# Start addresses of the matmul operands moved to multiples of 512 bytes, in a gated-attention kernel with two expert layers

## The chip, the core and the metric

The kernel runs on one core of a Trainium2 chip. The metric is device time in microseconds (us) of one execution, as the median of several; lower is better. The core has TensorE (PE, matmuls), VectorE (DVE), ScalarE (ACT), GpSimd (POOL), and SyncE (SP), whose queue issues the DMAs here. On-chip memory (SBUF) has 128 partitions, and a tensor in it starts at the same byte address in each of them; matmul results go to PSUM, in eight banks.

## The reference

A gated linear attention makes x, a bilinear layer follows, then a mixture of four experts:

```
state = alpha[t][:, None] * state + k[t] (outer) v[t];  y[t] = q[t] @ state      # 4 batches, 8 heads, 768 steps, D = 48
x = y as [3072 tokens, 384]
x = ((x @ w1) * (x @ w2)) @ w3 @ w_out                                           # 384 -> 1024 -> 384
p = domain_probs / (sum(domain_probs) + 1e-9)
out = sum over e of p[:, e] * (relu(x @ w1e[e]) @ w2e[e])                        # 4 experts, 384 -> 1024 -> 384
```

## The kernel before

Matrices are float32. A product is made from three float32r matmuls: each operand is split into a high part (a copy rounded to float32r, by ACT) and a low part (what the rounding left, by DVE or POOL), and high*high, high*low and low*high are added in PSUM. The program has three stages.

The fold (from the start to about 60 us) multiplies w3 by w_out once, `wp = w3 @ w_out`, with plain float32 matmuls of 384 columns (lines 1132 and 1147), while the first chunks of the attention are worked on beside it.

The bilinear stage (about 60 to 430 us) runs over 4 batches, two tiles of 384 tokens in each and 8 steps of 128 features in a tile. A step makes `a` and `b` from the tile `x0` and the weights `wb` (`up1`), multiplies them to `g` (DVE), and adds `g @ wp` into three PSUM banks (`down1`); all of it goes through `split_product` (lines 940 to 942), which is 27 matmuls of 384 columns in a step and 1728 in the stage. Its moving operand (the one that is streamed, the other being loaded into the array beforehand) is `x0`, read as three pieces of 128 columns that lie 4096 bytes apart, or `g`, read as one piece. Beside the steps, PE works on the attention of the next chunk (`visit`), DVE prepares the one after it, and SP moves data: the keys are turned by way of memory (`keys_spill`, lines 312 and 320) and a part of x0 is moved between partitions (`move_rest`, line 355), for which PE waits on `x0_moved` before the first step of a tile. The result `x1` is written to memory.

The expert stage (about 430 to 1230 us) is 4 experts times 3 rounds times 16 steps, 192 steps. A step is 9 matmuls of 512 columns (`up2_product`, line 1089: moving `x1`, loaded `we`) laid among 12 of 384 columns (`down2_product`, line 1198: moving `we`, loaded `h`), 4032 matmuls in the stage with a few less at its edges. ACT writes `h_hi` and DVE `h_lo` from the PSUM bank that a step filled, two steps ahead of their use.

The order on every engine is written out by hand, and waits are on semaphores.

SBUF tensors are laid out one behind the other, in the order in which the program names them (the helper `sb`); each starts at the next multiple of 32 bytes, and the first of the kernel's own at byte 1152. Tensors named with the context `first` are given back at `first.close()`, and those behind it (x1, we1, total) start again where the first of them (`inputs`) did. So these starts follow:

| tensor | role in the matmuls | start before (bytes) | over a multiple of 512 | start after | over |
|---|---|---|---|---|---|
| h_hi, h_lo | loaded, line 1198 | 3552, 7648 | 480 | 4096, 8192 | 0 |
| x1 tiles (four) | moving, line 1089 | 11968 and on | 192 | 12288 and on | 0 |
| inputs | attention | 11968 | 192 | 12288 | 0 |
| keys_t, values | attention | 46784, 40640 | 192 | 47104, 40960 | 0 |
| decayed, scores | attention | 49600, 50656 | 448, 480 | 49920, 50944 | 256 |
| wb, we1 (and low) | loaded or moving | 54752 and on | 480 | 55296 and on | 0 |
| wp (and low) | loaded, `down1` | 103904 and on | 480 | 104448 and on | 0 |
| x0 tiles (two) | moving, `up1` | 128480, 140768 | 480 | 129024, 141312 | 0 |
| a, g (and parts) | moving (g) | 153056 and on | 480 | 153600 and on | 0 |
| we0, w3 | loaded or moving | 174560 | 480 | 175104 | 0 |

Slices of the weights that a matmul reads start at multiples of 512 bytes from the tensor's start. Every start is a multiple of 32 bytes, before and after; those at 192 are multiples of 64 too, those at 480 are not.

Of the kernel before, what the change touches and what calls it, by code (L numbers as in the profile page):

```python
# [24 lines left out]
F32 = mybir.dt.float32  # L25
F32R = mybir.dt.float32r
# [4 lines left out]
P = 128  # L31
BATCH, HEADS, SEQ, D = 4, 8, 768, 48
CHUNK = P
CHUNKS = SEQ // CHUNK
PAIRS = HEADS // 2
# [8 lines left out]
KT, FT = DM // P, FF // P  # L44
# [9 lines left out]
TILE2 = 512  # L54
# [24 lines left out]
TURNED = CHUNKS - 1  # L79

ATTENTION_COLUMNS = (SLOTS * 3 + 2 + 2 + 2 + 1) * PAIRS * CHUNK + SLOTS * VD + PAIRS * P + PAIRS * D + PAIRS * ODD + 2 * PAIRS
ATTENTION_REST = ATTENTION_COLUMNS - 4 * KT * TILE2
REDO_X0 = 2 * CHUNKS


def gated_attention_experts(nc, akq, v, akq_long, v_columns, w3T, w_out, wsets, probs, out):
# [4 lines left out]
    with ExitStack() as ctx:  # L91
        def sb(name, shape, dt=F32, where=ctx):
            return where.enter_context(nc.sbuf_tensor(name, shape, dt))
# [13 lines left out]
        gate = sb("gate", [P, TOKENS // P, EXPERTS])  # L107
        gate_sum = sb("gate_sum", [P, TOKENS // P])
        gate_inv = sb("gate_inv", [P, TOKENS // P])
        h_hi = sb("h_hi", [P, 2, TILE2], F32R)  # L110
        h_lo = sb("h_lo", [P, 2, TILE2], F32R)
        outside = sb("outside", [PD, BATCH * CHUNKS])
        outside_sum = sb("outside_sum", [1, 1])
        regular = sb("regular", [1, 1], mybir.dt.int32)
        head_sum = sb("head_sum", [PD, 2])
        alpha_range = sb("alpha_range", [PD, 2])


        first = ExitStack()
# [7 lines left out]
        keys_t = sb("keys_t", [P, PAIRS, P], F32, first)  # L127
        state = sb("state", [PD, PAIRS, D], F32, first)
        decayed = sb("decayed", [PD, PAIRS, ODD], F32, first)
        chunk_decay_inv = sb("chunk_decay_inv", [PD, 2, PAIRS], F32, first)  # L130
        scores = sb("scores", [P, 2, PAIRS, CHUNK], F32, first)

        wb_hi = sb("wb_hi", [P, WSET], F32R, first)
        raw = ExitStack()
# [27 lines left out]
        for slot in range(2):  # L162
            x1_hi[slot] = sb(f"x1_{slot}_hi", [P, KT, TILE2], F32R)
            x1_lo[slot] = sb(f"x1_{slot}_lo", [P, KT, TILE2], F32R)
        sb("attention_rest", [P, ATTENTION_REST])
        we_hi[1] = sb("we1_hi", [P, WSET], F32R)
# [1119 lines left out]
```

## Time and profile before

| | |
|---|---|
| median of 3 runs | 1230.63 us (1230.1 to 1231.71) |
| the profiled execution's own time | 1231.72 us |
| its span (first to last instruction) | 1230.0 us |
| mean granted TensorE clock | 1.00 of full speed |
| busy: PE, PEld, DVE, ACT, POOL | 99%, 91%, 36%, 22%, 14% of the span |
| DMA | 107.49 MB, 87 GB/s over the span |

PE is the matmul side of TensorE, PEld the loading of its stationary operand. Matmuls are pipelined: the record of one lasts longer than the distance to the next one's start, so the cost of a matmul in a stream is read as the distance between starts, or as a stretch divided by the matmuls that start in it. The queue of SP is shown as SPq.

### The profile page before, as it was taken

To read this page: it belongs to the slowest core of one execution; us is meant where nothing else is said; L and a number is where in the kernel's file an instruction comes from. 1 tells how busy PE (TensorE), PEld (TensorE's weight loads), DVE (VectorE), ACT (ScalarE), POOL (GpSimd) and SP (SyncE) were. 2 spreads that over 40 slices of the span, in tenths; PEclk is the share of its full clock that TensorE was granted. 3 is DMA by queue.
4 is the path that set the end of the run, shared out by engine and by line. 5 is a ranking of instruction groups with operands and counts; after the bars stand their busy time and mean duration, and the time that the engine had idled before them with its cause. 6 is when DMAs were issued, how large, how long until landed. Compare 5 with 4: busy or idle time off the path is not lost.

```text
span 1230.0 us, 18716 instructions
## 1 busy us (share of the span) xinstructions
PE 1218.8 (99%) x7714; PEld 1114.2 (91%) x7714; DVE 446.6 (36%) x873; ACT 276.0 (22%) x515; POOL 168.1 (14%) x148
## 2 busy tenths in 40 slices
PE   9998999999999999999999999999999999999999
PEld 6698999999999999999999999999999999999998
DVE  4876765765741122222222222221222222222222
ACT  1433333333332321111111111111111111111111
POOL 1122222222222630000000000000000000000000
PEclk9999999999999999999999999999999999999999
DMA  9634635635622440111141111113011111222201
GB/s 274 214 77 106 144 104 121 144 106 119 139 58 110 142 166 28 51 51 52 52 155 52 52 51 51 52 51 132 25 50 51 52 52 52 78 77 77 77 4 48
DMA packets 81639, 107.49 MB, mean 87 GB/s; under 512 B 36001, under 2 KB 54689, under 8 KB 81057
## 3 DMA queue, kind: packets, MB, share of 16 engines
q1 hardware_dynamic: 81568, 106.50, 28.9%
q8 instruction: 51, 0.84, 0.3%
q14 instruction: 20, 0.16, 0.1%
HBM read 86.03 MB, written 18.09 MB: 85 GB/s over the span
## 4 chain that ended last, share of the span: by engine, by line
PE 91%; DVE 4%; DMA 2%; SPq 2%; issue 1%; ACT 1%; DVEq 0%; ACTq 0%
PE bank L1089 32%; PE bank L1198 24%; PE score_banks L1198 8%; PE bank L940 7%; PE bank L942 6%; PE bank L941 6%; PE bank L1132 2%; PE bank L1147 1%; PE bank L979 1%; PE bank L989 1%; DMA keys_t<-keys_spill 1%; PE score_banks L1000 1%; SPq L320 1%; DMA keys_spill<-key_blocks 1%; DVE suffix L687 1%; PE score_banks L965 1%
## 5 line engine op out<-in xcount | busy, mean ns | idle before, releaser
L764 DVE SCALAR_TENSOR_TENSOR h_lo<-bank,h_hi 128x512 fp32r<-128x512 f32 x192 | 132.7, 691 | 584.7 <-ACT h_hi L558 583.8
L558 ACT ACTIVATE h_hi<-bank 128x512 fp32r<-128x512 f32 x192 | 114.7, 597 | 661.4 <-PE bank L1089 661.4
L1089 PE MATMUL bank<-x_hi,we_lo 128*128 128x512 f32 x576 | 228.7, 397 | 0.0
L1089 PE MATMUL bank<-x_hi,we_hi 128*128 128x512 f32 x576 | 224.1, 389 | 0.0
L1089 PE MATMUL bank<-x_lo,we_hi 128*128 128x512 f32 x576 | 223.5, 388 | 0.0
L1198 PE MATMUL bank<-we_hi,h_hi 128*128 128x384 f32 x576 | 194.6, 338 | 0.0
L1198 PE MATMUL bank<-we_lo,h_hi 128*128 128x384 f32 x576 | 194.5, 338 | 0.0
L1198 PE MATMUL bank<-we_hi,h_lo 128*128 128x384 f32 x576 | 193.8, 336 | 0.0
L461 POOL TENSOR_TENSOR we_lo<-we_raw,we_hi (+1 forms) x48 | 60.9, 1291 | 527.6 <-ACT we_hi L519 527.6
L940 PE MATMUL bank<-x,wb_hi 128*128 128x384 f32 x384 | 128.8, 335 | 3.6 <-DMA x<-x 2.3
L1089 PEld LDWEIGHTS bank<-x_lo,we_hi 128*128 128x128 f32 x576 | 108.3, 188 | 22.7
L1089 PEld LDWEIGHTS bank<-x_hi,we_lo 128*128 128x128 f32 x576 | 108.3, 188 | 22.4
L942 PE MATMUL bank<-x,wb_lo 128*128 128x384 f32 x384 | 128.4, 334 | 0.0
L941 PE MATMUL bank<-x,wb_hi 128*128 128x384 f32 x384 | 128.3, 334 | 0.0
L1198 PEld LDWEIGHTS bank<-we_hi,h_lo 128*128 128x128 f32 x576 | 108.3, 188 | 8.5
L1198 PEld LDWEIGHTS bank<-we_hi,h_hi 128*128 128x128 f32 x576 | 108.3, 188 | 8.4
L1089 PEld LDWEIGHTS bank<-x_hi,we_hi 128*128 128x128 f32 x576 | 108.3, 188 | 0.2
L1198 PEld LDWEIGHTS bank<-we_lo,h_hi 128*128 128x128 f32 x576 | 108.1, 188 | 0.0
L471 POOL TENSOR_TENSOR g_lo<-g_sb,g_hi 128x384 fp32r<-128x384 f32 x64 | 65.5, 1023 | 233.2 <-ACT g_hi L548 233.2
L940 PEld LDWEIGHTS bank<-x,wb_hi 128*128 128x128 f32 x384 | 72.1, 188 | 4.7 <-DMA x<-x 2.9
L754 DVE TENSOR_TENSOR g_sb<-a_sb,bank 128x384 f32<-128x384 f32 x64 | 35.2, 551 | 105.6 <-PE bank L942 103.0
L941 PEld LDWEIGHTS bank<-x,wb_hi 128*128 128x128 f32 x384 | 72.1, 188 | 0.0
(89 smaller groups left out, 1434.8 us busy)
## 6 DMA issues: line engine op xcount, KB each, us to landing
x_hi<-x_hi_spill SPq DMA_DIRECT2D x24, 768.0 KB, 4.8
x_lo<-x_lo_spill SPq DMA_DIRECT2D x24, 768.0 KB, 6.4
inputs<-akq SPq DMA_DIRECT2D x24, 672.0 KB, 5.5
we_raw<-wset SPq DMA_DIRECT2D x4, 3072.0 KB, 10.1
values<-v_rows SPq DMA_DIRECT2D x24, 256.0 KB, 5.8
x_hi_spill<-x_hi_out SPq DMA_DIRECT2D x8, 576.0 KB, 3.4
x_lo_spill<-x_lo_out SPq DMA_DIRECT2D x8, 576.0 KB, 4.4
keys_spill<-key_blocks SPq DMA_DIRECT2D x60, 64.0 KB, 1.8
```

Of the source, the lines that this page charges most:

```text
L320: sp.dma_start(keys_t[:, pair, :].rearrange("p (i e) -> p i e", i=BLOCKS), rows[:, :, pair * BLOCK:(pair + 1) * BLOCK]).then_inc(keys_t_lo ...
L461: pool.tensor_tensor(set_lo(n)[:, at], set_raw(n)[:, at], set_hi(n)[:, at], ALU.subtract).then_inc(piece_lo, 1)
L471: pool.tensor_tensor(g_lo[:, s % 2, :], g_sb[:, s % 2, :], g_hi[:, s % 2, :], ALU.subtract).then_inc(g_lo_ready, 1)
L558: act.activation(h_hi[:, s % 2, :], bank[s % 2][:, :], ACT.Relu).then_inc(h_hi_ready, 1)
L754: dve.tensor_tensor(g_sb[:, s % 2, :], a_sb[:, s % 2, :], bank[1][:, 0:TILE1], ALU.mult).then_inc(g_ready, 1)
L764: dve.scalar_tensor_tensor(out=h_lo[:, s % 2, :], in0=bank[s % 2][:, :], scalar=0.0, in1=h_hi[:, s % 2, :], op0=ALU.max, op1=ALU.subtract) ...
L940: pe.matmul(dst, left[0], right[0], start=first, stop=False)
L941: pe.matmul(dst, left[0], right[1], start=False, stop=False)
L942: return pe.matmul(dst, left[1], right[0], start=False, stop=last)
L1089: mm = pe.matmul(bank[s % 2][:, :], (we_hi if term < 2 else we_lo)[e % 2][:, cols], (x1_lo if term == 1 else x1_hi)[u][:, k, :], start=(i ...
L1132: mm = pe.matmul(bank[FOLD_BANKS[f]][:, 0:DM], w3_sb[:, k, f * P:(f + 1) * P], wo_sb[:, k, :], start=(k == 0), stop=(k == FT - 1))
L1198: mm = pe.matmul(bank[SUM_BANKS[sub]][:, 0:DM], (h_hi if term < 2 else h_lo)[:, s % 2, rows], (we_lo if term == 1 else we_hi)[e % 2][:, cols],
```

## The change

Two tensors that nothing reads are put in as padding, `edge_of_h` (320 bytes in each partition) and `edge_of_weights` (224 bytes). h_hi and h_lo are named behind the five small tensors that they stood ahead of, and `chunk_decay_inv` (32 bytes) behind `scores`. `attention_rest`, the space kept between x1 and we1, is 224 bytes longer so that we1 still lies on wb. Every instruction, wait, shape and DMA, and the order on each engine, is the same as before; only addresses in SBUF differ. All tensors of the table move; the highest byte used in a partition goes from 223712 to 224256.

```diff
 ATTENTION_COLUMNS = (SLOTS * 3 + 2 + 2 + 2 + 1) * PAIRS * CHUNK + SLOTS * VD + PAIRS * P + PAIRS * D + PAIRS * ODD + 2 * PAIRS
-ATTENTION_REST = ATTENTION_COLUMNS - 4 * KT * TILE2
+EDGE_OF_H, EDGE_OF_WEIGHTS = 80, 56
+ATTENTION_REST = ATTENTION_COLUMNS + EDGE_OF_WEIGHTS - 4 * KT * TILE2
...
         gate_inv = sb("gate_inv", [P, TOKENS // P])
-        h_hi = sb("h_hi", [P, 2, TILE2], F32R)
-        h_lo = sb("h_lo", [P, 2, TILE2], F32R)
         outside = sb("outside", [PD, BATCH * CHUNKS])
...
         alpha_range = sb("alpha_range", [PD, 2])
+        sb("edge_of_h", [P, EDGE_OF_H])
+        h_hi = sb("h_hi", [P, 2, TILE2], F32R)
+        h_lo = sb("h_lo", [P, 2, TILE2], F32R)
...
         decayed = sb("decayed", [PD, PAIRS, ODD], F32, first)
+        scores = sb("scores", [P, 2, PAIRS, CHUNK], F32, first)
         chunk_decay_inv = sb("chunk_decay_inv", [PD, 2, PAIRS], F32, first)
-        scores = sb("scores", [P, 2, PAIRS, CHUNK], F32, first)
+        sb("edge_of_weights", [P, EDGE_OF_WEIGHTS], F32, first)
```

## Rows read from the trace of the kernel before

**Rows 1.** The page's head: busy time of each engine over the span.
```profile
span 1230.0 us, 18716 instructions
PE 1218.8 (99%) x7714; PEld 1114.2 (91%) x7714; DVE 446.6 (36%) x873; ACT 276.0 (22%) x515; POOL 168.1 (14%) x148
```

**Rows 2.** Windows; columns: stretch, length, engines, granted clock, DMA share, GB/s.
```profile
60.00:150.00 90.00, 84.56 (x832) 80.56 (x831) 66.09 (x150) 31.00 (x64) 23.54 (x21) 1.00 0.44 101
250.00:350.00 100.00, 99.06 (x920) 95.77 (x919) 63.77 (x144) 33.51 (x68) 25.86 (x24) 1.00 0.48 114
600.00:800.00 200.00, 200.00 (x1012) 182.31 (x1011) 47.53 (x73) 34.91 (x60) 15.23 (x12) 1.00 0.18 63
```

**Rows 3.** Timeline of PE, expert stage, one step; columns: start, record's length, instruction.
```profile
700.13 0.39 PE L1089 MATMUL bank<-x_hi,we_hi 128*128 128x512 f32 x1
700.36 0.34 PE L1198 MATMUL bank<-we_hi,h_hi 128*128 128x384 f32 x1
700.54 0.39 PE L1089 MATMUL bank<-x_lo,we_hi 128*128 128x512 f32 x1
...
704.29 0.39 PE L1089 MATMUL bank<-x_hi,we_hi 128*128 128x512 f32 x1
```

**Rows 4.** Timeline of PE, bilinear stage: first with g, then with x0 moving.
```profile
299.53 0.33 PE L941 MATMUL bank<-g_lo,wp_hi 128*128 128x384 f32 x1
...
300.40 0.33 PE L940 MATMUL bank<-x,wb_hi 128*128 128x384 f32 x1
...
303.17 0.33 PE L941 MATMUL bank<-x,wb_hi 128*128 128x384 f32 x1
```

**Rows 5.** The chain that ended last, in the fold: start, length, what.
```profile
19.35 3.24 PE bank L1132 x10
22.60 0.59 PE score_banks L965 x14
```

**Rows 6.** Groups of PE by line and shape: busy us, mean ns of one record, idle.
```profile
L1089 PE MATMUL bank<-x_hi,we_lo 128*128 128x512 f32 x576 | 228.7, 397 | 0.0
L1089 PE MATMUL bank<-x_hi,we_hi 128*128 128x512 f32 x576 | 224.1, 389 | 0.0
L1089 PE MATMUL bank<-x_lo,we_hi 128*128 128x512 f32 x576 | 223.5, 388 | 0.0
...
L1198 PE MATMUL bank<-we_hi,h_hi 128*128 128x384 f32 x576 | 194.6, 338 | 0.0
...
L942 PE MATMUL bank<-x,wb_lo 128*128 128x384 f32 x384 | 128.4, 334 | 0.0
...
L941 PE MATMUL bank<-g_lo,wp_hi 128*128 128x384 f32 x192 | 64.2, 334 | 0.0
```

**Rows 7.** Waits of PE for other engines and DMAs: us in total, times, longest.
```profile
PE score_banks L965 <- DMA keys_t<-keys_spill: 3.0, 4, 1.5
PE bank L940 <- DMA x<-x: 2.3, 1, 2.3
PE bank L940 <- DVE g_sb L754: 1.3, 1, 1.3
```

**Rows 8.** The chain that ended last, up to the longest of these waits.
```profile
100.23 1.80 DMA keys_spill<-key_blocks
...
104.17 1.66 SPq L320
...
105.87 2.24 SPq L355
...
108.15 2.22 DMA x<-x
...
110.41 0.44 PE bank L940
```

**Rows 9.** DMA issues: count, KB each, median us to landing.
```profile
x_hi<-x_hi_spill SPq DMA_DIRECT2D x24, 768.0 KB, 4.8
...
keys_t<-keys_spill SPq DMA_DIRECT2D x60, 64.0 KB, 4.5
...
x<-x SPq DMA_DIRECT2D x48, 48.0 KB, 2.8
```

## The prediction

> **What bounds the kernel.** I read the page's head first: PE is busy 99% of a span of 1230.0 us, DVE 36%, ACT 22% [rows 1]. A busy PE can still stand in line for data, so next come the waits of PE: all that it waited for others is 3.0 + 2.3 + 1.3 = 6.6 us, 0.5% of the span [rows 7]. The windows say the same by stage: 200.00 busy of 200.00 among the experts, 99.06 of 100.00 in the bilinear stage, 84.56 of 90.00 between 60 and 150 us, all at a granted clock of 1.00, which is the 2.4 GHz level [rows 2]. So the kernel is a stream of matmuls, and a change that leaves every instruction in place can act in two ways only: on the distance between the starts of two matmuls, or on those 6.6 us of waits (with small stalls behind them, which add little).
>
> **What a matmul costs.** In the expert stage a step goes from 700.13 to 704.29, 4.16 us for 9 matmuls of 512 columns and 12 of 384 [rows 3]. After a start with 512 columns the next comes 0.23 us later, after one with 384 0.18 us later: 128 columns more cost some 0.05 us, one column in each cycle at 2.4 GHz. By that rate the columns of a step take 9 x 213.3 + 12 x 160 = 3840 ns, and 4160 - 3840 = 320 ns is on top, 15 ns for each of 21 matmuls. The window gives the same: 200 us over 1012 starts is 197.6 ns, the columns are 3840 / 21 = 182.9, 14.7 ns on top [rows 2]. In the bilinear stage, with x0 moving, 16 distances take 303.17 - 300.40 = 2.77 us, 173.1 ns each, 13 on top of 160; with g moving 5 take 0.87 us, 174 each, 14 on top [rows 4]. The float32 matmuls of the fold start 10 times in 22.60 - 19.35 = 3.25 us, 325 ns each (the step to the next kind counted in); that is two cycles for each column, 320, and at most 5 ns on top [rows 5]. So a float32r matmul pays 13 to 15 ns beyond its columns, a float32 one 5 or less. Over 1728 + 4032 matmuls this is 1728 x 13 + 4032 x 14.7 = 82 us. That is all that the operands' addresses could possibly have to do with on PE, and it is what has to be judged.
>
> **The change part by part.** It removes and adds no instruction and moves none past another, so each part is a new address and its price is what that address does.
>
> (a) The moving operand. Before there were three cases. x1 stood 192 bytes over a multiple of 512; we and g 480 over; x0 480 over too, but read in three pieces, so it would meet a bad start three times where g meets it once. They cost the same: x0 13 ns, g 14 ns on top [rows 4], and the mean records of x0 and g are both 334 ns [rows 6]. x1, with 64-byte alignment, has 230 - 213 = 17 ns behind it at the two digits of the timeline, and no less than we has [rows 3]. If a start off 512 cost one more fetch, three pieces would pay three times; they pay nothing. Price taken: 0. From both sides: at best the 13 to 15 ns fall to the 5 ns of the fold (a gain of 8 x 1728 + 9.7 x 4032 = 53 us), at worst a matmul pays what separates the dearest row of its kind from the cheapest, 397 - 388 = 9 ns (rival 3). I take 0 because the nearest rows, x0 against g, differ in just what would matter and agree.
>
> (b) The loaded operand (h, we, wb, wp). All of these stood 480 over before, 32 bytes off a multiple of 64, so no row here shows an aligned one. This is the weak place. What speaks for 0: the time on top is the same 13 to 15 ns under 384 and under 512 columns [rows 3, 4], so it isn't a load that ends too late, which 53 ns more of columns would cover. What speaks against: float32 loads stood 480 over too (w3) and show 5 ns or less [rows 5], but there the columns take twice as long and could hide a loss. Price taken: 0, with the same ends as in (a).
>
> The Trainium skill, "SBUF — State Buffer" (box on SBUF cachelines in the section on the DMA port swizzle), says that engines read lines of 16 bytes. All starts before and after are multiples of 16, so by that rule nothing changes on PE, though it leaves the 13 ns unexplained and no row here shows such a line.
>
> (c) DVE, ACT, POOL. Their operands move in the same way. DVE matters only from 60 to 110 us, where it is behind part of the chain; over the span it has 64% of slack [rows 1]. Nothing in the trace ties its times to an address. 0.
>
> (d) DMAs. Their SBUF ends move from 192 or 480 over to 0. Only two kinds are waited for: keys_t, 3.0 us in four waits, and x<-x, 2.3 us in one [rows 7]. In the longest wait, the chain runs through a spill of 1.80 us, the queue of SP (1.66 us and 2.24 us are two of its pieces) and an x<-x of 2.22 us [rows 8], so about 4 us of 10 are transfers. Most of such a transfer is not data: 48 KB land after 2.8 us where 768 KB land after 4.8 [rows 9], so (768 - 48) KB cost 2.0 us and 48 KB of data only 0.13 us, the rest being fixed. Were the data part of the transfers a fifth cheaper, a chain of two or three would gain under 0.1 us; with keys_t in four waits I take 0.3 us in all. The ends: 0, and all 5.3 us of waits for DMA gone; and +1 us if the order of landings falls worse. The ends of x1, we and inputs are hidden: PE has no wait for them in the list.
>
> The Trainium skill, "DMA: Bandwidth & Descriptors" (How a descriptor splits into AXI transactions), speaks for a gain: a piece that doesn't start at a multiple of 256 bytes fetches from the boundary below it. By it a 1024-byte piece of x0 at 480 over costs 39 beats, and 32 at 0, an estimate of 18% less; on the 0.13 us of data that is 0.02 us, on a whole landing of 2.2 us 0.4 us. No row here has an aligned DMA to hold against it, and the sum above goes without it.
>
> **The sum.** 0 on PE, 0.3 us less on DMA waits. The profiled execution took 1231.72 us for a span of 1230.0, 1.7 us around it, and lies 1.1 us above the median of 1230.63. Taken from its own time, 1231.7 - 0.3 = 1231.4; against the median, 1230.3. I give 1230.3.
>
> **The rivals.**
> 1. The time on top is an alignment loss of float32r, and it goes. All of it down to the fold's 5 ns gives 1230.6 - 53 = 1177; if only the loaded operand counts in one of the two kinds, or half is left, about 1204. For it: float32 matmuls don't have it [rows 5], and no loaded operand was aligned. Against it: x0 in three pieces equals g in one [rows 4, 6], and x1 at 192 is no better than we at 480 [rows 3]. A loss that comes only from the loading side is still open. Chance 0.12.
> 2. The waits for DMA shrink enough to be seen: more than 2.5 us of their 5.3. Their whole goes to 1225.3; half gives 1228. For it: the transfers stand on the chain [rows 8]. Against: they are mostly fixed time [rows 9], and SP's queue stands between them. Chance 0.05.
> 3. Slower: two reads, or a read and a write, in step. Before, x1 stood 192 over and h and we 480 over, so that the up matmul's stream and the load of the next h beside it began in different places modulo 512; afterwards all begin in the same. Where such a meeting costs time, line 1089 shows it: its third kind already has a record of 397 ns against 388 and 389 for the others [rows 6], at the same shape, so something does cost 8 to 9 ns there. If the other two kinds take that price, 2 x 576 x 8.5 = 10 us are added, 1240. Against: x0 with wb, and we with h, were in step before (all 480 over) and have the lowest times on top. It decides from the mean of those two rows: at 392 it would be some 4 us. Chance 0.09.
> 4. Something slower of 2.5 us or more from the early part, DMA landings that fall worse for SP's queue: the waits of [rows 7] grow by half, 1233.9. Chance 0.04.
> The forecast, no change, has 0.70. That the change doesn't do what it says is no rival here: the starts in the table follow from the sizes of the tensors.
>
> **How the numbers follow.** The bound of 0.2% is 2.5 us, about what a measurement of this kernel can tell from no change; three runs lay 1.6 us apart. Faster is rivals 1 and 2, 0.17; slower rivals 3 and 4, 0.13; same 0.70. The forecast's own range is 1228.2 to 1233.1. To leave out no more than 2 in 10 the range takes in rival 2 down to its end, 1225, and rival 3 up to 1240; what is left out is mostly rival 1 (0.12), which lies far below.
>
> **What would show it.** In the profile after: a step of the expert stage again 4.16 us long, and 1012 starts in 600 to 800 us, one more or less; if rival 1 holds, 1012 becomes above 1030 and the distances of 173 ns fall toward 165. Line 1089's three rows should stay at 397, 389 and 388; rival 3 lifts the lower two. The bilinear window should keep its 920 starts. The waits of PE should be 6.6 us within 1 us, with x<-x still there. I am wrong if the distance between float32r matmuls moves by as little as half a nanosecond: over 5760 of them that is 2.9 us.

## The result, and the profile after

The kernel after takes 1244.15 us (median of 5, 1243.47 to 1245.33) against 1230.1 us before (5, 1228.65 to 1231.71); the ratio of the runs on record is 1.0102, 95% interval 1.0086 to 1.0118 (the two medians alone give 1.0114, inside it). It is slower by 1%. The forecast was 1230.3 us, no change, with a range up to 1240: it was wrong. The span went from 1230.0 to 1241.9 us.

The page of the kernel after, its head:

```profile
span 1241.9 us, 18716 instructions
PE 1232.7 (99%) x7714; PEld 1119.0 (90%) x7714; DVE 446.3 (36%) x873; ACT 276.1 (22%) x515; POOL 168.2 (14%) x148
```

PE alone has grown, 1218.8 to 1232.7 us; DVE, ACT and POOL are the same within 0.3 us [rows 1]. The window of the expert stage in the kernel after (columns as in [rows 2]):

```profile
600.00:800.00 200.00, 200.00 (x993) 180.16 (x992) 44.95 (x69) 34.31 (x59) 15.28 (x12) 1.00 0.18 63
```

Among the experts 993 matmuls fit where 1012 did [rows 2], at the same granted clock of 1.00. The timeline of PE in the kernel after shows a step from 700.65 to 704.89, 4.24 us, against 4.16 [rows 3]; line 1092 is line 1089 of before:

```profile
700.65 0.39 PE L1092 MATMUL bank<-x_hi,we_hi 128*128 128x512 f32 x1
700.88 0.34 PE L1201 MATMUL score_banks<-we_hi,h_lo 128*128 128x384 f32 x1
701.06 0.40 PE L1092 MATMUL bank<-x_lo,we_hi 128*128 128x512 f32 x1
701.29 0.34 PE L1201 MATMUL bank<-we_hi,h_hi 128*128 128x384 f32 x1
...
704.89 0.39 PE L1092 MATMUL bank<-x_hi,we_hi 128*128 128x512 f32 x1
```

What is loaded beside each stream is in the same timeline, in the rows of PEld:

```profile
700.65 0.19 PEld L1201 LDWEIGHTS score_banks<-we_hi,h_lo 128*128 128x128 f32 x1
700.88 0.19 PEld L1092 LDWEIGHTS bank<-x_lo,we_hi 128*128 128x128 f32 x1
701.06 0.19 PEld L1201 LDWEIGHTS bank<-we_hi,h_hi 128*128 128x128 f32 x1
```

A load starts together with the matmul before its own: at 700.65 and 701.06 x1 is streamed and h is loaded, at 700.88 the weights are streamed and weights are loaded. Where two down matmuls follow each other, the weights are streamed and h is loaded. In a step of this order no weights are loaded beside a stream of x1.

The groups of PE after (mean ns of a record before the last bar):

```profile
L1092 PE MATMUL bank<-x_hi,we_lo 128*128 128x512 f32 x576 | 229.2, 398 | 0.0
L1092 PE MATMUL bank<-x_lo,we_hi 128*128 128x512 f32 x576 | 229.2, 398 | 0.0
L1092 PE MATMUL bank<-x_hi,we_hi 128*128 128x512 f32 x576 | 224.6, 390 | 0.0
...
L1201 PE MATMUL bank<-we_hi,h_hi 128*128 128x384 f32 x576 | 195.5, 339 | 0.0
...
L945 PE MATMUL bank<-x,wb_lo 128*128 128x384 f32 x384 | 128.4, 334 | 0.0
```

The row of x_lo went from 388 to 398 ns, the level that x_hi,we_lo had already; the others rose by 1; the bilinear rows stayed at 334 [rows 6]. Records hide part of it, distances between starts do not. Their means over the stage's steps, worked out from all starts in the two traces (D a down matmul of 384 columns, U0, U1, U2 the up matmuls with x_hi,we_hi, with x_lo and with we_lo):

| from > to | D>D | D>U0 | U0>D | D>U1 | U1>D | D>U2 | U2>D | sum, x 3 = a step |
|---|---|---|---|---|---|---|---|---|
| before, ns | 174.2 | 175.0 | 226.7 | 180.0 | 225.8 | 172.5 | 232.5 | 4160 |
| after, ns | 175.8 | 181.7 | 229.2 | 175.8 | 237.5 | 175.8 | 237.5 | 4240 |

They repeat to 1 ns from step to step, but for a few distances where the stage begins and ends, whichever of four experts, three values of k and eight of f the matmul is for. So nothing random is at work in these two kernels, and nothing that hangs on where in a tensor a matmul reads, which changes in steps of 512 bytes or more. Nor is it the writing of h: ACT and DVE write it in 0.6 and 0.7 us of a step's 4.2, while the distances are alike in all three thirds of a step. The two ends of the stage, first from the timeline of before, then of after:

```profile
426.42 0.39 PE L1089 MATMUL bank<-x_hi,we_hi 128*128 128x512 f32 x1
...
1226.57 0.34 PE L1198 MATMUL bank<-we_hi,h_lo 128*128 128x384 f32 x1
```

```profile
423.20 0.39 PE L1092 MATMUL bank<-x_hi,we_hi 128*128 128x512 f32 x1
...
1238.53 0.34 PE L1201 MATMUL bank<-we_hi,h_lo 128*128 128x384 f32 x1
```

The expert stage takes 815.33 us instead of 800.15, 15.2 us more, which is 192 steps of 79 ns. It begins 3.2 us earlier. 15.2 - 3.2 = 12.0, the growth of the span. These are two single executions, and single ones of one kernel lie 2 to 3 us apart; with the medians the kernel lost 14.05 us, so the early part gave back 1.1 us of the 15.2, and with the recorded ratio 2.7 us (0.7 to 4.6 by its interval). The waits of PE after, against [rows 7], hold 2.1 of the 3.2 us:

```profile
PE score_banks L968 <- DMA keys_t<-keys_spill: 1.8, 1, 1.8
PE bank L943 <- DMA x<-x: 1.4, 1, 1.4
PE bank L943 <- DVE g_sb L757: 1.3, 1, 1.3
```

### The profile page after: what moved, and what is told of

Read it like the earlier page. It is cut to its first block, busy times and chain, and to the rows that moved or that the text cites. A ratio compares the mean times of both kernels' runs of the same rounds, so it can differ in the third digit from the quotient of the medians.

```text
span 1241.9 us, 18716 instructions
## 1 busy us (share of the span) xinstructions
PE 1232.7 (99%) x7714; PEld 1119.0 (90%) x7714; DVE 446.3 (36%) x873; ACT 276.1 (22%) x515; POOL 168.2 (14%) x148
## 4 chain that ended last, share of the span: by engine, by line
PE 95%; DVE 3%; SPq 1%; DMA 1%; ACT 0%; issue 0%; DVEq 0%
PE bank L1092 33%; PE bank L1201 25%; PE score_banks L1201 8%; PE bank L943 8%; PE bank L945 7%; PE bank L944 7%; PE bank L1135 2%; PE bank L982 2%; PE bank L1150 1%; PE score_banks L1003 1%; PE bank L992 1%; PE score_banks L968 1%; DVE wb_lo L773 0%; DVE suffix L690 0%; DVE decay L711 0%
## 5 line engine op out<-in xcount | busy, mean ns | idle before, releaser
L1092 PE MATMUL bank<-x_hi,we_lo 128*128 128x512 f32 x576 | 229.2, 398 | 0.0
L1092 PE MATMUL bank<-x_lo,we_hi 128*128 128x512 f32 x576 | 229.2, 398 | 0.0
```

The source lines that it names most:

```text
L1092: mm = pe.matmul(bank[s % 2][:, :], (we_hi if term < 2 else we_lo)[e % 2][:, cols], (x1_lo if term == 1 else x1_hi)[u][:, k, :], start=(i ...
```

## The experiments

Theory A: the price depends on how x1 stands to h and to the weights modulo some length. Theory B: it depends on each start by itself. All kernels but the two named up384, which leave out a quarter of the tokens of the expert stage, compute the whole result. x1_224 and x0_g_224, taken on two chips with the same starts of x1, h and the weights, have the same seven distances to 0.1 ns, so one profile of a kernel is enough for those; it is not enough for 1 or 2 us in the whole time. Each of the first group is the kernel after with other paddings; `edge_of_x1` is a third padding, between h_lo and the attention's inputs:

```diff
-EDGE_OF_H, EDGE_OF_WEIGHTS = 80, 56
+EDGE_OF_H, EDGE_OF_X1, EDGE_OF_WEIGHTS = 80, 56, 0        # x1_224; all_480: 72, 0, 56; h_w_288: 24, 56, 0
...
         h_lo = sb("h_lo", [P, 2, TILE2], F32R)
+        sb("edge_of_x1", [P, EDGE_OF_X1])
```

**all_480.** 

> h, x1 and the weights all start 480 bytes over a multiple of 512 (before: h and weights 480, x1 192; after: all 0). Theory A, in step: what costs the 80 ns in each expert step (4.16 to 4.24 us) is that x1 now starts at the same place modulo 512 as h and the weights, wherever that is. It expects this kernel to be like the one after: 992 or 993 matmul starts in 600 to 800 us, some 1244 us. Theory B, the place itself: weights or h at 0 over are dear and at 480 over cheap. It expects 1012 starts and some 1230 us.

Measured: 1246.5 us, ratio to before 1.0126 (1.0108 to 1.0143), a step of 4.24 us, and each of the seven distances as after, within 0.1 ns. Its window:

```profile
600.00:800.00 200.00, 200.00 (x993) 180.14 (x992) 45.64 (x69) 34.32 (x59) 15.30 (x12) 1.00 0.17 59
```

None of x1, h and the weights starts at a multiple of 64 bytes in it. Theory B falls for h and the weights, which stand where they stood before. That x1's own start could be dear, at 480 as at 0, is not excluded here; h_w_288 below does that, with x1 at 0 and a step of 4.16 us.

**x1_224.** 

> The kernel after, with x1 (and the attention's inputs, which share its start) moved 224 bytes further, so that x1 stands to the weights and h as it did before, but these stay at 0 over. Theory A (only the relation counts): 1012 starts in 600 to 800 us, a step of 4.16 us, 1230 us. Theory B (weights and h at 0 are dear by themselves): 993 starts, 4.24 us, 1244 us.

Measured: 1230.47 us, ratio 0.999 (0.998 to 1.0), 4.16 us a step, the seven distances those of before. One tensor's place undoes the whole loss.

```profile
600.00:800.00 200.00, 200.00 (x1011) 182.20 (x1010) 47.77 (x73) 34.91 (x60) 15.23 (x12) 1.00 0.18 63
```

**The other places of x1.** One profile and one time each (0 and 224 are the kernels above, with their medians). The attention's tensors, which are not in use in the expert stage, move along.

> As x1_224 but x1 only 32 bytes over, weights and h at 0. 224 and 32 are the same modulo 64. Theory A with a period of 64 bytes: the same as x1_224, 4.16 us a step. Theory A with a longer period: a third value. Theory B: 4.24 us.

> As x1_224 but x1 64 bytes over, weights and h at 0. Theory A with a period of 64 bytes or less: like the kernel after, 4.24 us a step, 993 starts. With a longer period: some other value, perhaps 4.16. Theory B: 4.24 us.

> The kernel after, x1 at 128 over, weights and h at 0. With x1 at 32, 64 and 224 over the step was 4.17, 4.18 and 4.16 us. A fixed loss only where the starts are equal expects 4.16 to 4.18 here; a loss that repeats every 128 bytes expects 4.24.

> The kernel after, x1 at 256 over, weights and h at 0. The steps were 4.24 (0), 4.17 (32), 4.18 (64), 4.19 (128) and 4.16 us (224). A loss that repeats every 256 bytes expects 4.24; one that fades with the distance expects 4.16 to 4.18.

> The kernel after, x1 at 96 over, weights and h at 0. Theory P: the loss has a period of 256 bytes and one peak, at equal starts (4.24 us at 0 and 256), and is flat elsewhere: 4.16 to 4.19 us a step. Rival Q: it also has peaks between, in which case some of 96, 160 and 192 reach 4.2 or more. For the bilinear stage: it has ended at 422 to 424 us wherever the attention's inputs started at 0, 32, 64, 128 or 256 over and at 425 or later at 192, 224 and 480; I expect 424 here.

> As x1_96, x1 at 160 over. Theory P: 4.16 to 4.19 us a step. Rival Q: 4.2 or more at one of the three. Bilinear stage: 425 if the late end goes with starts in the upper half of 256 bytes, else 423.

> As x1_96, x1 at 192 over. This differs from x1_224 (4.16) by one step of 32 bytes. Theory P: 4.16 to 4.18 us a step. Rival Q: 4.2 or more at one of the three. Bilinear stage: 426, as before, where the inputs stood at 192 too.

Measured, with h and weights at 0 over (the step is the trace's distance over ten steps, divided by ten):

| x1 over 512 | 0 (after) | 32 | 64 | 96 | 128 | 160 | 192 | 224 | 256 |
|---|---|---|---|---|---|---|---|---|---|
| step, ns | 4240 | 4170 | 4180 | 4200 | 4190 | 4200 | 4200 | 4160 | 4240 |
| U1>D, ns | 237.5 | 230.0 | 232.5 | 231.5 | 234.2 | 232.5 | 231.6 | 225.8 | 237.5 |
| whole time, us | 1244.15 | 1230.64 | 1231.99 | 1235.57 | 1235.23 | 1237.26 | 1237.16 | 1230.47 | 1242.62 |
| first up matmul at, us | 423.2 | 423.5 | 423.0 | 422.7 | 424.3 | 424.4 | 424.3 | 426.6 | 422.2 |

At 256 all seven distances are those of 0: a shift by 256 bytes changes nothing there, and each smaller shift does. Whether the other places repeat 256 bytes on was not tried. In x1_32 and x1_128 the distances change in turn from step to step (4168 and 4172, 4186 and 4194 ns), and the table has the means. Equal starts are the dearest place, 40 ns above the next, but the rest isn't flat: the expected 4.16 to 4.19 was too narrow, three places have 4.20, which just meets what rival Q asked. The kernel of before stood, by chance or not, at the best of the eight. The first up matmul, expected at 424, 423 or 425, and 426 us for 96, 160 and 192 over, came at 422.7, 424.4 and 424.3.

**h_288 and w_288.** 

> The kernel after, with h_hi and h_lo alone moved, to 288 over a multiple of 512, so that x1 stands 224 bytes past h modulo 512 as it did before; x1 and the weights stay at 0 over. Theory A1: what counts is the stream of x1 in an up matmul against h, which is loaded beside it for the next down matmul; a step of the expert stage falls back to about 4.16 us, span some 1230. Theory A2: what counts is x1 against the weights; the step stays at 4.24 us. Something between means that both count.

> The kernel after, with all weights, x0 and g moved together to 288 over, so that x1 stands 224 bytes past the weights as before; h and x1 stay at 0 over. Theory A1 (x1 against h): 4.24 us a step. Theory A2 (x1 against the weights): 4.16. It also sets h against the weights for the first time: what the down matmuls pay for being in step would show as another distance between two down matmuls (175.8 ns after, 174.2 before).

Measured: 4220 and 4200 ns (1239.12 and 1236.31 us, one time each). Neither kernel gives back all of the 80 ns: one gives 20, the other 40. D>D, where no x1 takes part, went from 175.8 to 175.0 and 176.7. But each of these kernels also moves h against the weights, by 224 bytes one way or the other, which theories A1 and A2 leave out: of the three differences between x1, h and the weights two fix the third. So they don't show that x1 against the weights counts by itself. By the rows of PEld above, x1 meets h and the weights meet h, but x1 and the weights never meet in these steps, and a step that depends on x1 to h and h to the weights alone fits all the runs as well. No run decides between the two.

**h_w_288.** 

> h and all weights (with x0 and g) at 288 over, x1 and the attention's inputs at 0 over: all relations modulo 512 among x1, h and weights are those of before, while the attention's inputs start at a multiple of 512. Theory A (only relations count on PE) expects a step of 4.16 us with the very distances of before, one by one: 174.2, 175.0, 226.7, 180.0, 225.8, 172.5, 232.5 ns. In h_288 and w_288, where one relation each was set back, the step was 4.22 and 4.20, so both must be needed. The bilinear stage ended at 423.4 us in w_288 against 426.4 before; if that comes from the inputs' start, it does so here too, and the kernel takes 1227 to 1228 us, 0.2% less than before. If the early gain was chance, 1230.

Measured: 4160 ns, the seven distances all as expected to 0.1 ns, with x1 at 0 over and no start where it was before. So the differences between the starts decide in the expert stage, not the starts. The kernel takes 1229.7 us (median of 12) against 1231.18 for before on the same chip, ratio 0.9983 (0.9969 to 0.9996): 0.2% less than before, as expected, though the time itself lies nearer to 1230 than to 1227 or 1228, and by the two ratios 1.2% less than after. Its expert stage takes 800.15 us, to the digit what it took before, and begins 3.7 us earlier in the profiled execution, which was the fastest of the 12 (1228.02 us); by the medians the gain is 1.5 us. The two ends of the stage:

```profile
422.73 0.39 PE L1092 MATMUL bank<-x_hi,we_hi 128*128 128x512 f32 x1
...
1222.88 0.34 PE L1201 MATMUL bank<-we_hi,h_lo 128*128 128x384 f32 x1
```

**x0_g_224.** Two more paddings, 224 bytes ahead of x0 and 288 behind x1_lo_out. 

> x1_224, with x0, a and g also moved, to 224 over, while wb and wp stay at 0 over: the first kernel in which the bilinear stage's streamed and loaded operands don't start in step. If being in step costs there what it costs among the experts, the distance of 173 ns falls by a few ns and the stage gets shorter by up to 1728 x 4 ns = 7 us; if the loss needs 512 columns or two kinds of matmul in turn, it stays at 173 ns. The expert stage as in x1_224, 4.16 us a step.

Measured: the bilinear distances stay at 173 ns, the expert step at 4.16 us, 1230.44 us. So 224 bytes between x0 or g and their weights change nothing in the bilinear stage; other distances were not tried.

**up384_after and up384_before.** Why not, then?

```diff
-mm = pe.matmul(bank[s % 2][:, :], ..., (x1_lo if term == 1 else x1_hi)[u][:, k, :],
+mm = pe.matmul(bank[s % 2][:, 0:384], ..., (x1_lo if term == 1 else x1_hi)[u][:, k, 0:384],
...
-rows = slice(sub * P, (sub + 1) * P)
+rows = slice(sub % 3 * P, (sub % 3 + 1) * P)
```

> The layout after, with the up matmuls of the expert stage cut from 512 to 384 columns; the fourth part of each tile of 512 tokens is left out and the first taken again in its place, ACT and DVE work on 384 columns of h. All addresses that a matmul starts from are those of the kernel after. If the loss comes with the in-step starts alone, the 21 matmuls keep it and a step is 21 x 173.3 = 3640 ns plus most of the 80 ns that after lost against before. If it needs streams of different lengths in turn (so that the loads drift against the streams), the distances are 173 to 174 ns throughout, as in the bilinear stage, and a step is 3.64 us.

> The same cut of the up matmuls to 384 columns in the layout of before. With up384_after it gives the difference of the two layouts at equal lengths: 80 ns a step if the addresses alone decide, 0 if the loss needs unequal lengths, in which case both stand at 3.64 us.

Measured: in up384_after every distance is 173.3 ns (3640 a step), in the layout that cost most at 512 columns. All six groups of the stage have records of 334 ns, as in the bilinear stage; two of them:

```profile
L1092 PE MATMUL bank<-x_lo,we_hi 128*128 128x384 f32 x576 | 192.4, 334 | 0.0
...
L1201 PE MATMUL bank<-we_hi,h_lo 128*128 128x384 f32 x576 | 192.4, 334 | 0.0
```

up384_before takes 3660: the order of the two layouts is turned round. It has distances of 170.0 and 180.0 ns among others of 173 to 175. So of the two layouts the one with equal starts is the better while all streams have 384 columns; the addresses alone don't decide, nor do equal lengths alone bring the difference to 0, as one of the theories had it. Why 224 bytes cost 20 ns a step here and nothing in the bilinear stage stays open.

**The grouped kernels.** A step's 12 down matmuls first, then its 9 up matmuls:

```diff
-                ups = 0
                 for i in range(SUBS * TERMS):
                     down2_product(e, m, s, i)
-                    if ahead and i % SUBS >= 1:
-                        up2_product(ahead[0], ahead[2], ups)
-                        ups += 1
+                if ahead:
+                    for i in range(KT * TERMS):
+                        up2_product(ahead[0], ahead[2], i)
```

> The layout after (all starts at 0 over), with the matmuls of a step in the expert stage no longer laid among each other: first the 12 down matmuls of 384 columns, then the 9 up matmuls of 512. All else as in the kernel after. Theory C: in step is harmless, even best, while streams of one length follow each other (bilinear stage 173 ns, up384_after 173.3 ns), and costs where 384 and 512 take turns. It expects 173.3 and 226.7 ns, 13.3 over the columns in both, with a loss only at the two changes, so 4.12 to 4.13 us a step: 192 x 0.115 = 22 us less than after, 1222 us, below the kernel before. Rival theory D: any stream of 512 columns in step with its loads costs 237.5 ns, whatever follows: a step of 12 x 173.3 + 9 x 237.5 = 4.22 us, 1240.

> The same grouping in the layout of before (x1 192 over, h and weights 480 over). Theory C with only the alternation at fault expects 4.12 to 4.13 us here too, 1224 us. If the relation of x1 to the weights has a price of its own in a run of up matmuls, the distance between two of them shows it (up384_before had 173.3 to 175.5, and 179.9 between two down matmuls), and a step is up to 4.16 us.

> The grouping with x1 at 64 over, h and weights at 0. Together with grouped_after (0) and grouped_before (224 apart) it shows whether the distance between two up matmuls depends on how x1 stands to the weights. Theory C expects 226.7 ns in all three; if the relation has a price in a uniform run too, the three differ.

Measured: grouped_after has 4187 ns a step and 1233.51 us, ratio to before 1.0013 (1.0001 to 1.0025); grouped_before 4173 ns, 1235.09 us, 1.0025 (1.0013 to 1.0038), with its expert stage starting at 428.9 us; grouped_x1_64 4173 ns, 1232.59 us. Theory C (4.12) and theory D (4.22) both fail. Grouping takes 53 ns from a step in the layout after and adds 13 in the layout before. What the steps of grouped_after show, here where a run of up matmuls gives way to one of down matmuls:

```profile
701.00 0.39 PE L1092 MATMUL bank<-x_hi,we_lo 128*128 128x512 f32 x1
701.23 0.33 PE L1201 MATMUL score_banks<-we_hi,h_hi 128*128 128x384 f32 x1
...
701.75 0.35 PE L1201 MATMUL bank<-we_hi,h_hi 128*128 128x384 f32 x1
701.93 0.34 PE L1201 MATMUL bank<-we_lo,h_hi 128*128 128x384 f32 x1
702.11 0.34 PE L1201 MATMUL bank<-we_hi,h_lo 128*128 128x384 f32 x1
702.29 0.33 PE L1201 MATMUL bank<-we_hi,h_hi 128*128 128x384 f32 x1
...
703.16 0.33 PE L1201 MATMUL bank<-we_hi,h_lo 128*128 128x384 f32 x1
703.33 0.39 PE L1092 MATMUL bank<-x_hi,we_hi 128*128 128x512 f32 x1
```

The mean distances of the 12 down matmuls in a step are 170.8, 175.0, 177.5, 185.0, 175.8, 181.7 ns, and then six times 173.3: after the change of length the stream needs some six matmuls (702.29 in the rows) to find the steady 173.3, which costs 26 ns in all. The 9 up matmuls never settle: 224.2 to 235.8, mean 231.2, where 226.7 would be the columns and 13.3, so 41 ns a step. In grouped_before the change costs only 3 ns, over three matmuls, and the up matmuls have a mean of 232.2, 50 ns in all; in grouped_x1_64 it is 25 ns over seven matmuls and a mean of 229.8, 28 ns. So there are two losses, one at a change of length and one within runs of 512 columns, both differ with the starts, and neither follows the other. That the first is what alternating lengths pay all the time is likely, and not shown by itself.

## Why the prediction was wrong

**The stream of matmuls as the bound.** Right. PE was and is busy 99%, and nothing but the distances and the early part moved. Two readings in it were loose. The view of PE's waits has a fourth row that I left out, 1.2 us for `ones` at the start, the same before and after. And the fold's 80 records on line 1132 come from 40 matmuls of the program, two for each, so "5 ns or less" holds for a record, half a float32 matmul.

**Part (a), the moving operand, price 0.** This is the step that failed. I held x0 in three pieces against g in one, and x1 against we, to see whether a bad start costs something by itself. It doesn't: all_480 confirms that. But I made from it that addresses cost nothing, while the rows of x0 and g both stood in step with their weights and came from a stage with one length of stream. The question was the relation, and only rival 3 asked it. What the runs showed in its place: with all starts equal the distances of the expert stage rise by 3.8 ns on average, U1>D from 225.8 to 237.5 ns, a step from 4160 to 4240 ns and the stage by 15.2 us, and x1_224 takes all of it back by moving x1 alone. The worst end that I gave in (a), 9 ns for a matmul, covers the mean of 3.8 and not U1>D, which rose by 11.7. The reading that x1 has "no less than we" behind it was beyond what two digits tell (17 against 20 ns); the means of all distances are 15.0 and 15.4 ns over the columns.

**Part (b), the loaded operand, price 0.** The weak place named there was not the one that gave. An aligned start of the loaded operand brings nothing (x1_224: weights and h at 0 over, 4.16 us), and the bilinear distances with x0 moving have a mean of 173.4 ns in all twenty profiles, so rival 1 falls, and with it the hope of 53 us. What counts is how h, the weights and x1 stand to each other (h_288, w_288, h_w_288).

**Part (c), 0.** Right: the times of DVE, ACT and POOL by group are the same within 2 ns for all the large groups.

**Part (d), DMAs, 0.3 us.** The direction was right and the size too small: 3.2 us between the two profiles, 1.1 by the medians, 2.7 by the ratio. The waits for DMA fell from 5.3 to 3.2 us, and x<-x from 2.3 to 1.4. I allowed for the data part of two or three transfers and took the fixed part as fixed. The median landing of keys_t moved by far more than that, from 4.5 us [rows 9] to 4.1, while x<-x went from 2.8 to 2.7 and the spill of the keys stayed at 1.8:

```profile
keys_t<-keys_spill SPq DMA_DIRECT2D x60, 64.0 KB, 4.1
...
x<-x SPq DMA_DIRECT2D x48, 48.0 KB, 2.7
```

It goes with the start of keys_t, which moves with the attention's inputs: 4.1 to 4.3 us in the seven profiles with that start at a multiple of 256 bytes, 4.3 at 128 over, and 4.5 to 4.8 in the twelve others. The early end goes with the start of the inputs more roughly: the first up matmul came at 422.2 to 424.8 us in the thirteen profiles with that start at 0 to 160 over 256 bytes, and at 424.3 to 428.9 in the seven others. But single profiles of one start differ by as much (192 over: 424.3, 425.1, 426.4, 428.9), my expectations for 96 and 192 over were off by 1.3 and 1.7, and the stage ended early (423.5, 423.0) in x1_32 and x1_64 too, where keys_t took 4.7 us. So keys_t can't be all of it; what else gives the gain was not separated. The 0.02 to 0.4 us that the prediction worked out for one x<-x finds no support in its 0.1 us.

**Rival 3, chance 0.09, 1240 us.** This is what happened, in kind: x1, h and the weights begin in the same place, the third kind of up matmul keeps its 397 ns, and x_lo rises to it. In size it was 15 us on PE and not 10: it counted the records of two rows, of which only one rose, and left out that the distances of 384 columns move too. Its own test, the mean of the two lower rows, came out at 394, which by its scale is 6 us: records understate what distances lose. The argument that I held against it, that operands in step had the lowest times, was true (up384_after) and did not carry over to streams of 512 and 384 columns in turn. The two rows of 397 and 388 ns at one shape were the sign that a relation has a price; a chance of 0.09 did not do them justice.

**The signs that I named.** The step was to stay at 4.16 us and came to 4.24, 1012 starts became 993, and the waits of PE were to be 6.6 us within 1 and came to 4.5. Half a nanosecond in the distances was to prove me wrong, and they moved by 3.8. The 920 starts between 250 and 350 us became 980, but that says nothing of the distances: more of the attention's short matmuls (514 starts instead of 448) fall in that window, and the distances with x0 moving are 173.4 ns in both.

**What lies behind the relation.** By the Trainium skill, "SBUF — State Buffer" (box on SBUF cachelines), with its lines of 16 bytes, nothing should have changed on PE; every start was a multiple of 32 bytes and a step grew by 80 ns, so the measurement decides: the rule is not enough to predict a stream. The Trainium skill, "TensorE: Matmul & The Clock Gate" (What happens when you issue a matmul, its step on LDWEIGHTS), says that loading the next weights takes no read bandwidth from the running matmul, as the two have ports of their own. The runs show that the distance between float32r matmuls depends on how the starts of the operands stand to each other, which that rule does not provide for. That the reads of load and stream meet in SBUF is the explanation I would give; the pairs that the rows of PEld show fit it, but no run measured a meeting, and it stays argued. Why 256 bytes, and why runs of 512 columns don't settle where 384 do, is open.

## What to carry to other kernels

Where matmuls bound a kernel, read the distance from start to start to the nanosecond for each kind, and treat the start addresses of streamed and loaded operands, relative to each other, as a parameter to be tried in steps of 32 bytes over 256: here eight places of one tensor spanned 4160 to 4240 ns a step, 1.2% of the kernel, with no instruction changed. Round numbers are no safe choice: all at multiples of 512 was the worst place tried, together with all at 480 over. A rule drawn from one stage (one length of stream) must not be carried to a stage that mixes lengths without a row from there.

## What the runs showed of the hardware that I had not expected

With x0 moving, the float32r matmuls of 384 columns in the bilinear stage start 173.4 ns apart on average in all twenty profiles, and those of up384_after 173.3: the columns at 2.4 GHz (granted clock 1.00) and 13.3 ns. With up matmuls of 512 columns in the expert stage every layout paid more on average, at best 15.2 ns over the columns (4160 ns a step). Moving x1 by 256 bytes left all seven distances as they were, each smaller shift changed them. The disturbance at a change from 512 to 384 columns lasts six or seven matmuls and costs 25 ns with h and the weights at 0, and is almost absent (3 ns) in grouped_before. A step of 21 matmuls came out at a whole multiple of 10 ns in every layout in which the two kinds alternate (4160 to 4240, and 3640 and 3660 with 384 columns), in x1_32 and x1_128 as the mean of two steps. A DMA of 64 KB into keys_t landed after 4.1 to 4.3 us where its start there was a multiple of 256 bytes, and after 4.5 to 4.8 us at 32, 64, 96, 160, 192 and 224 over.
